# Attention scores from q and k split into a rounded part and a low part, three fp32r products in place of plain fp32 matmuls

## What is computed

```python
def _attn_ref(q, k, v, M_prev, z_prev, beta):
    scores = scale * np.matmul(q, k.transpose(0, 1, 3, 2))
    scores = np.where(causal, -1000000000.0, scores)
    a = np.exp(scores - scores.max(-1, keepdims=True))
    a /= a.sum(-1, keepdims=True) + 1e-09
    local = np.matmul(a, v)
    ...
    return (g * mem_out + (1 - g) * local).astype(np.float32)

def reference(**kwargs):
    ...
    x = _moe_ref(x=x, **moe_kwargs)     # (x @ w_in), ELU, @ w_out
    return _moe2_ref(x=x, **moe2_kwargs)  # (x @ w_in), h * relu6(h + 3) / 6, @ w_out
```

## Time and profile before

| | us |
|---|---|
| median of three runs | 1121.03 (1120.95 to 1123.28) |
| the profiled execution | 1122.92 |
| its span | 1121.1 |
| TensorE busy | 1076.2 (96%) |
| DVE busy | 677.8 (60%) |
| ACT busy | 298.4 (27%) |
| GpSimd busy | 192.5 (17%) |

### The profile page before, as it was taken

How to read it: one execution, slowest core, us unless ns; L and a number is a source line. 1 busy time by engine, 2 the same in 40 slices (tenths; PEclk the granted TensorE clock), 3 DMA queues, 4 the chain that set the end, 5 groups by cost and what they waited for, 6 DMA issues and landing times.

```text
span 1121.1 us, 16386 instructions
## 1 busy us (share of the span) xinstructions
PE 1076.2 (96%) x6080; PEld 966.3 (86%) x6080; DVE 677.8 (60%) x1278; ACT 298.4 (27%) x737; POOL 192.5 (17%) x202
## 2 busy tenths in 40 slices
PE   5999999999889999999999999899999999999998
PEld 2667676676879999999999999898999999899997
DVE  5676766767388544545454468865656565565654
ACT  3666666666432212112121123301001010000100
POOL 3434434344265000000000025500000000000000
PEclk9999999999889999999999999999999999999999
DMA  4322121220134000000000014100000000000000
GB/s 162 119 97 101 52 101 56 98 101 20 38 113 132 1 1 1 0 0 0 0 0 0 0 37 131 57 1 13 15 0 28 0 28 0 0 28 0 28 0 28
DMA packets 16599, 44.56 MB, mean 40 GB/s; under 512 B 1968, under 2 KB 1968, under 8 KB 16560
## 3 DMA queue, kind: packets, MB, share of 16 engines
q1 hardware_dynamic: 16560, 44.05, 11.3%
HBM read 39.33 MB, written 4.72 MB: 39 GB/s over the span
## 4 chain that ended last, share of the span: by engine, by line
PE 89%; DVE 6%; issue 3%; ACT 1%; DMA 1%; SPq 0%; DVEq 0%
PE ps L473 35%; PE ps L494 18%; PE ps L486 17%; PE ps L450 8%; PE ps L384 3%; DVE pt_lo L751 2%; PE ps L379 1%; PE ps L459 1%; PE ps L428 1%; PE ps L418 1%; PE ps L387 1%; DVE x_all L795 1%; ACT r_rows L570 1%; PE ps L405 1%; DVE h_hi L824 1%
## 5 line engine op out<-in xcount | busy, mean ns | idle before, releaser
L473 PE MATMUL ps<-x_hi,w 128*128 128x384 f32 x1536 | 392.5, 336 | 0.0
L473 PEld LDWEIGHTS ps<-x_hi,w 128*128 128x128 f32 x1536 | 280.9, 189 | 7.4
L473 PE MATMUL ps<-x_lo,w 128*128 128x384 f32 x768 | 258.3, 336 | 0.0
L486 PE MATMUL ps<-h_hi,w 128*128 128x384 f32 x768 | 196.6, 336 | 6.0 <-DVE h_lo L826 6.0
L494 PE MATMUL ps<-w,h_hi 128*128 128x512 f32 x576 | 179.2, 392 | 3.1 <-DVE h_lo L826 3.1
L824 DVE CAST h_hi<-act_tmp 128x384 fp32r<-128x384 f32 x192 | 108.9, 567 | 100.9 <-PE ps L486 53.2
L486 PEld LDWEIGHTS ps<-h_hi,w 128*128 128x128 f32 x768 | 139.5, 189 | 7.0 <-DVE h_lo L826 7.0
L473 PEld LDWEIGHTS ps<-x_lo,w 128*128 128x128 f32 x768 | 144.7, 188 | 0.0
L296 POOL TENSOR_TENSOR w<-stage,w 128x1024 f32 (+1 forms) x32 | 77.7, 2436 | 358.3 <-ACT w L544 358.3
L486 PE MATMUL ps<-h_lo,w 128*128 128x384 f32 x384 | 129.0, 336 | 0.0
L494 PEld LDWEIGHTS ps<-w,h_hi 128*128 128x128 f32 x576 | 106.8, 188 | 22.1 <-issue 2.4
(11 more groups left out here) (110 smaller groups left out, 1233.8 us busy)
## 6 DMA issues: line engine op xcount, KB each, us to landing
nat<-nat_in SPq DMA_DIRECT2D x16, 768.0 KB, 5.4
qk<-qk_t SPq DMA_DIRECT2D x16, 608.0 KB, 3.8
stage<-w_in SPq DMA_DIRECT2D x32, 256.0 KB, 2.7
stage<-w_out SPq DMA_DIRECT2D x32, 256.0 KB, 2.9
out<-rows_out SPq DMA_DIRECT2D x18, 256.0 KB, 2.1
beta_sb<-beta SPq DMA_DIRECT2D x1, 4.0 KB, 6.5
```

The source lines that it names most:

```text
L473: mm = pe.matmul(ps[:, bank:bank + CHUNK], w[:, n, wp, 0, cols], xp[:, m, :], start=(m == 0 and part == 0), stop=(m == KM - 1 and part == 2))
L486: mm = pe.matmul(ps[:, Y_AT + 512 * m:Y_AT + 512 * m + CHUNK], w[:, n, wp, 1, cols], hp[:, n % 2, :], start=(n == 0 and part == 0), stop=( ...
```

## The change

`qk` is replaced by three tiles: `qk_raw`, one buffer, what the DMA brings; `qk_hi`, two buffers of type fp32r, written by GpSimd: q times -0.125 and k, rounded (two instructions in place of the one that scaled q); `qk_lo`, two buffers of type fp32r, written by DVE: what the rounding left, one `scalar_tensor_tensor` of 640 columns for q and one `tensor_tensor` of 576 columns for k. TensorE makes each score tile from three products: hi by hi, hi by lo, lo by hi.

TensorE waits for DVE's `qk_split` where it waited for `q_scaled`. SP loads the raw tile of pair p once pair p - 1 is split. GpSimd and DVE write the buffer of pair p once the scores of pair p - 2 are done. DVE splits pairs 0 and 1 ahead of the loop, on both sides of `phi_of_q(0)` and `gates()`, and pair g + 1 at the end of slot 4 of round g, for g from 1 to 14. (The lines with C2 and C3 in the diff compute the same index in another way.)

```diff
-    qk = sb("qk", [2, QCOLS + S])
+    qk_raw = sb("qk_raw", [QCOLS + S])
+    qk_hi = sb("qk_hi", [2, QCOLS + S], F32R)
+    qk_lo = sb("qk_lo", [2, QCOLS + S], F32R)
...
             def load_qk(p):
-                if p >= 2:
-                    sp.wait_ge(scores_done, QT * (p - 1))
-                sp.dma_start(qk[:, p % 2, :], qk_t[p]).then_inc(qk_loaded[p % 2], 16)
+                if p >= 1:
+                    sp.wait_ge(qk_split, p)
+                sp.dma_start(qk_raw[:, :], qk_t[p]).then_inc(qk_loaded, 16)
...
-            def scale_q(p):
-                u = p % 2
-                pool.wait_ge(qk_loaded[u], 16 * (p // 2 + 1))
-                pool.tensor_scalar(qk[:, u, 0:QCOLS], qk[:, u, 0:QCOLS], -0.125, 1.0, ALU.mult, ALU.mult).then_inc(q_scaled, 1)
+            def round_qk(p):
+                u = p % 2
+                pool.wait_ge(qk_loaded, 16 * (p + 1))
+                if p >= 2:
+                    pool.wait_ge(scores_done, QT * (p - 1))
+                pool.tensor_scalar(qk_hi[:, u, 0:QCOLS], qk_raw[:, 0:QCOLS], -0.125, 1.0, ALU.mult, ALU.mult).then_inc(qk_rounded, 1)
+                pool.tensor_scalar(qk_hi[:, u, QCOLS:QCOLS + S], qk_raw[:, QCOLS:QCOLS + S], 1.0, 1.0, ALU.mult, ALU.mult).then_inc(qk_rounded, 1)
...
                 if s == 0:
-                    pe.wait_ge(q_scaled, p + 1)
+                    pe.wait_ge(qk_split, p + 1)
                 if n >= 2:
                     pe.wait_ge(exp_done, n - 1)
+                parts = ((qk_hi, qk_hi), (qk_hi, qk_lo), (qk_lo, qk_hi))
                 if i == LAST:
                     at = last_at(n)
                     for lo, hi in ((0, S // 2), (S // 2, S)):
-                        pe.matmul(ps[:, at + lo:at + hi], qk[:, u, EDGE:QCOLS], qk[:, u, QCOLS + lo:QCOLS + hi], start=True, stop=(lo == 0))
+                        for part, (q, k) in enumerate(parts):
+                            pe.matmul(ps[:, at + lo:at + hi], q[:, u, EDGE:QCOLS], k[:, u, QCOLS + lo:QCOLS + hi], start=(part == 0),
+                                      stop=(part == 2 and lo == 0))
...
-                for a in range(2):
-                    at, d = score_at(n, a), slice(D * a, D * a + D)
-                    pe.matmul(ps[:, at:at + WIDTH[i]], qk[d, u, P * i:P * i + P], qk[d, u, QCOLS:QCOLS + WIDTH[i]], start=True, stop=False)
+                for part, (q, k) in enumerate(parts):
+                    for a in range(2):
+                        at, d = score_at(n, a), slice(D * a, D * a + D)
+                        pe.matmul(ps[:, at:at + WIDTH[i]], q[d, u, P * i:P * i + P], k[d, u, QCOLS:QCOLS + WIDTH[i]], start=(part == 0), stop=False)
...
+            def split_qk(p):
+                u = p % 2
+                hi = qk_hi.bitcast(F32)
+                dve.wait_ge(qk_rounded, 2 * p + 2)
+                if p >= 2:
+                    dve.wait_ge(scores_done, QT * (p - 1))
+                dve.scalar_tensor_tensor(out=qk_lo[:, u, 0:QCOLS], in0=qk_raw[:, 0:QCOLS], scalar=-0.125, in1=hi[:, u, 0:QCOLS],
+                                         op0=ALU.mult, op1=ALU.subtract)
+                dve.tensor_tensor(qk_lo[:, u, QCOLS:QCOLS + S], qk_raw[:, QCOLS:QCOLS + S], hi[:, u, QCOLS:QCOLS + S], ALU.subtract).then_inc(qk_split, 1)
...
+            split_qk(0)
             phi_of_q(0)
             gates()
+            split_qk(1)
             for g in range(PAIRS + 1):
...
+                    if s == 4 and 1 <= g < PAIRS - 1:
+                        split_qk(g + 1)
                     if s == 3 and g + 1 < PAIRS:
                         phi_of_q(g + 1)
```

More of the change, by code:

```diff
@@ L158, in semaphore @@
         return nc.alloc_semaphore(name)
-    qk_loaded = [semaphore(f"qk_loaded{i}") for i in range(2)]
+    qk_loaded = semaphore("qk_loaded")
     nat_loaded = [semaphore(f"nat_loaded{i}") for i in range(2)]
@@ L169, in build @@
     gate_exp = semaphore("gate_exp")
-    q_scaled = semaphore("q_scaled")
+    qk_rounded = semaphore("qk_rounded")
+    qk_split = semaphore("qk_split")
     scores_done = semaphore("scores_done")
@@ L339, in scale_phi @@
                 pool.tensor_tensor(ph, ph, f_nat[:, u, :].rearrange("p (x o) -> p x o", o=1).to_broadcast([P, 2 * QT, D]), ALU.mult).then_inc(phi_scaled, 1)
-            scale_q(0)
+            round_qk(0)
             pool.memset(prob[:, :, P_ALL - D:P_ALL], 0.0).then_inc(zeros_ready, 1)
@@ L346, in _ @@
                 if p == 0:
-                    scale_q(1)
+                    round_qk(1)
                 if p >= 1:
@@ L353, in _ @@
                 if 1 <= p < PAIRS - 1:
-                    scale_q(p + 1)
+                    round_qk(p + 1)
                 if p == 3:
@@ L413, in turn @@
                 elif c in (C2, C3):
-                    t = 2 + c - C2
+                    t = 2 if c == C2 else 3
                     for a in range(2):
```

## The result

The changed kernel takes 1187.1 us (median, 1186.6 to 1188.3) where the kernel before takes 1122.0 in the same comparison: 1.058 times the time, interval 1.056 to 1.060. The forecast was 1181.0, range 1155 to 1204, slower. The profiled execution took 1187.2 us, its span is 1185.4. The page of the changed kernel: busy time and granted TensorE clock in 40 slices, and the chain that ended last.

What follows compares the result with a forecast made beforehand. TensorE was taken to bound the kernel (89% of the chain). Wait 38.5, saving -3.6, start +2.0 and clock 23.1 sum to 60.0 us, from profiled 1122.9 to 1182.9, from median 1121.0 to the predicted 1181.0; range 1155 to 1204.

Steps and rivals of the forecast that it cites:

- The new wait: Wide scores wait for DVE's split at the end of slot 4: 2.75 us a pair, 14 times, 38.5 us.
- Fewer TensorE cycles: Score tiles as three fp32r products save TensorE 0.24 us a pair, 3.6 us over 15 periods.
- The heads overlap: In 64-row score tiles both heads' fp32r products run side by side; rival, one after the other: 1202 us, chance 0.11.
- The hole: After the 384-column scores TensorE waits 0.62 us for DVE's chunk split; savings in those scores are worth nothing.
- The start: DVE's two splits before the first maximum, one between the gates and it: +2.0 us, bounds 1 and 4.
- The clock: TensorE's granted clock falls after 7 of the 14 stalls, about 3.3 us each: 23.1 us, bounds 0 and 14 falls.
- The chances: Stall with 3 to 11 clock falls, 1166 to 1195 us: 0.62; 12 falls or more, 1195 to 1208: 0.07.

Runs made afterwards that it cites:

- The split in slot 3: Against the changed kernel, DVE's split of pair g+1 moved from the end of slot 4 to slot 3, ahead of `phi_of_q`: 1122.35 us.
- the comparison with the clock held: Two kernels with 13 filling matmuls before the wait for the split: plain fp32 scores 1157.4 us, three products 1153.7 us.
- the best of these kernels: Changed kernel with four further moves, the last making GpSimd's low weight part wait for `phi_of_q` of pair 4: 1112.05 us, 0.9915 of the kernel before.
- the order of slot 4: Against the kernel with the split in slot 3 (GpSimd waiting for pair 4's split), DVE's two phi splits precede the 128-column maximum: 1118.95 us.
- the later split of pair 1: Against the kernel with the new slot 4 order, DVE splits pair 1 behind the first two maxima, not ahead: 1115.7 us.
- GpSimd's wait: Against the kernel with pair 1's later split, GpSimd's low first weight tile waits for DVE's `phi_of_q` of pair 4, not its split: 1112.05 us.
- the kernel with half the split: Against the changed kernel, the q part of DVE's split moved to slot 3, the k part stayed at slot 4's end: 1165.3 us.

## Why the prediction was right or wrong

**The new wait: right.** The stall was to be 2.5 us by the records and is 2.45; from `phi_of_q` to the wide tile 3.91 was worked out and 3.88 measured. It came 14 times. A period with the clock whole was to be 19.9 (the prediction's own terms, 17.50 + 2.75 - 0.24, make 20.0) and is 19.80. The split in slot 3 removes it and leaves 1122.

**Fewer TensorE cycles: right in kind, a third too small.** I had 0.24 us a pair. The tiles show 0.09 + 0.16 + 0.08 - 0.06 = 0.27, and the wide tile another 0.07 when its weight load is covered (0.83), together 0.34; the comparison with the clock held gives 0.35. The spacings that I interpolated were 0.01 to 0.02 us too long at 288 and 256 columns (0.13 and 0.11) and 0.01 too short at 512 (0.23), and the fixed part of a tile, 0.22, was too much: 0.49 less three spacings of 0.11 leaves 0.16 for the 128-column tile. The heads overlap. Stall and saving together make 32.1 us (14 x 2.29) against the common period of before, 31.5 against its whole trace, where the prediction had 34.9.

**The hole hid more than I said.** The 384-column tile takes 0.72 us (156.57 to 157.29) where it took 0.85 (150.89 to 151.74 in the kernel before), and the wait behind it grew by as much, from 0.62 to 0.75, so its saving does go into the hole. What I missed is that the wide tile's saving too is worth nothing once the stall is gone, until DVE's order is changed: its end is followed by a chunk that waits for DVE.

**The start: wrong.** I had +2.0 us, bounds 1 and 4; the second wide tile is 0.2 us earlier than before. The failed step took the gates' end as fixed, with the first maximum at 15.11, and put the split behind it. DVE of the changed kernel:

```profile
9.97 0.17 DVE L738 COPY rest_by<-rest 64x4 f32<-64x4 f32 x1
...
12.58 2.14 DVE L781 SCALAR_TENSOR_TENSOR qk_lo<-qk_raw,qk_hi 128x640 fp32r<-128x640 f32 x1 [2.44 <-POOL qk_hi L307]
14.65 0.84 DVE L783 TENSOR_TENSOR qk_lo<-qk_raw,qk_hi 128x576 fp32r<-128x576 f32 x1
15.41 0.74 DVE L745 TENSOR_REDUCE neg_max<-ps 128x1 f32<-128x576 f32 x1
```

SP now issues pair 1's loads at 7.22, after the first split, and not at 2.14. The gates' own data is there sooner: ACT's first operation on beta starts at 6.54 in place of 8.22, and the gates begin at 8.37 in place of 9.92. And the later load of pair 1 holds GpSimd until 11.19, so DVE's gates, which in the earlier trace rows ran beside GpSimd's long operations (1.44 us for four elements), now run alone, and this copy ends at 10.14. Waiting for pair 1 and splitting it takes just the time that this frees. This is read from the two traces; no run moved the load alone.

**The clock: the mechanism right, the count wrong.** I had 7 falls at 3.3 us, 23.1 us; there were 12 at 2.8, 33.4 us. The count was a guess from two stretches, and taking half was the mis-sized term: a stall of 1.7 us already has 7 falls of 14, and the full one 12. The chances gave 3 to 11 falls 0.62 and 12 or more only 0.07, at 1195 us or above: the time fell into the range of the first, the count into the second. The total came out within 6 us because the start (2 us) and the stall with the saving (3 us) were too high where the clock (10 us) was too low. That they offset one another is luck.

The Trainium skill, page "TensorE: Matmul & The Clock Gate", section Why this matters for your kernels, advises against gaps above some 3 us. In these runs shorter ones were enough: the clock fell after 2.45 us and after 1.72 us.

**What stays open.** Which stretches make the clock fall is not settled. After 1.7 us it fell in 7 of 13 cases, after 2.46 us in 12 of 13 beside fp32r products and in 4 of 13 beside plain ones, in one trace each; the longest stall of each of the three kernels (2.76, 2.94 and 2.90 us, at pair 4) left it whole. That the plain matmuls' longer work around the stall makes the difference is a guess: no run varied that work alone, and the 2.07 us stretch of the feed-forward part, with the same work around it, fell in 5 traces of 12. So something besides the length and the neighbouring work decides, such as when the stretch comes; that was not tested.

## What to carry to other kernels

Before handing work to an idle engine, find the place in its list, and what the list waits for: with the same two DVE operations in slot 3, where DVE had idled, the kernel is 65 us shorter than with them at the end of slot 4. Price a recurring stall of TensorE twice, once as idle time and once for the clock after it; a run that fills the stall with useless matmuls separates the two. After a cheaper matmul form, look for what TensorE meets next, since here 0.25 of the 0.40 us a period came only with a new order on DVE, and the best of these kernels (0.99 of the time before) has four moves beside the products: the split in slot 3, the order of slot 4, the later split of pair 1 and GpSimd's wait.

## What the runs showed of the hardware that was not expected

**DVE and GpSimd exclude each other in some operations.** A DVE operation with two SBUF operands took 2.98 us in place of 0.82 beside a GpSimd operation of 2.38 us that had begun first; a one-operand fp32 operation took 2.64 in place of 0.50. In the earlier trace rows the latter takes 0.49, and GpSimd has no operation from 161 to 165 us there. Differences with an operand in PSUM were not slowed: DVE's splits of chunks took 0.69 us for 512 elements beside GpSimd's operations as well as alone. The Trainium skill, page "SBUF — State Buffer", section SBUF: two separate sides, says that of a DVE operation with two SBUF inputs (or in a two-port mode) and a GpSimd operation that reads SBUF, whichever starts first holds the shared ports for the whole instruction. The first row agrees: GpSimd's operation ended at 73.69, and DVE's 0.68 us later. So does the second (75.24, and 0.34 us later), if that operation is in such a mode, which no run shows.

**The clock can fall after 1.7 us of idle time.** In the kernel with half the split it did so 7 times in 13, for some 7 us each.

**The same idle stretch can cost the clock in one kernel and not in another.** The 2.07 us stretch of the feed-forward part was followed by a fall in 5 of 12 traces.

**A slower matmul form can be the faster kernel.** With the stall in place plain fp32 scores took 1172.3 us and the three products 1187.1, by the falls of the clock; with the clock held it was 1157.4 against 1153.7.
